# Two attention units of a batch in lockstep, in 64x32 and 32x64 tiles, with q, k, v read in long runs and the first phase's weights split on GpSimd

## The chip, the cores and the metric

One core of a Trainium2 chip runs the whole program in one launch. The metric is the device time of an execution in microseconds, the median over repeated runs. All inputs and outputs are float32 in HBM. TensorE (PE) multiplies, with its weight loads in a row of their own (PEld); VectorE (DVE), ScalarE (ACT) and GpSimd (POOL) do the rest; the DMA queues of SyncE (SP) and GpSimd bring the data.

## The reference

Three stages run one after the other, for a batch of 8 with 8 heads, 576 tokens and head width 64.

```python
def sm_attn(qq, kk, vv):                      # scale = 1/8
    s = scale * qq @ kk.T
    a = exp(s - max(s)); a = a / (sum(a) + 1e-9)
    return a @ vv
p_packed = sm_attn(p, k, v)                   # p: 32 rows per head
out      = sm_attn(q, p_packed, p_packed)     # 576 x 32 scores per head
x = out as (8, 576, 512)
# first phase: token shift, then
v = relu(xk @ w_k)**2 @ w_v ; r = sigmoid(xr @ w_r) ; x2 = r * v
# second phase: u = x2 + (x2.T @ U @ V).T ; result = u + relu(u @ w_ch1) @ w_ch2
```

## The kernel before

**Phases.** The 4608 rows of x are worked in two phases. In the first, four pairs of batches are done, each in three chunks of 384 tokens. A chunk has 17 slots (`SLOTS`): eight "k" slots (12 matmuls of 384 columns each, into `relu(x @ w_k)`), three "r" slots (12 matmuls of 512 columns) and six "v" slots (12 matmuls of 512 columns each). Each product is made in three passes over a high and a low float32r part, which ACT (high, a copy) and DVE (low, a subtraction) split off. In the second phase nine blocks of 512 tokens go through the 512 x 2048 x 512 network; the change leaves it alone.

**Attention.** A unit is four heads of a batch, so there are 16. A unit has ten steps ("k", "p", "scores1", "q", "a", "pv", "pp", "scores2", "norm", "out") that stand between the slots of the chunks. `chunk_plan` writes one list of items in order, and every engine and the SP queue walk that same list, each doing its own part of an item; so an engine that waits in one item does nothing of the next ones. `pair_units` says in which slot each step stands. The first pair works units 2 to 6 in its slots, the two middle pairs four units each (one hardware loop over both), the last pair one. Units 0 and 1 run before the first slot, in two sets of buffers, `main` and `side`, with the weights' staging between their steps (`first_items`).

**On the engines.** PE does two heads at a time: `scores1` and `scores2` are four matmuls of 288 columns with 128 rows and 64 output columns (L389, L417), because p and the packed result stand block-diagonally (`p_blk`, `pk_blk`, made with `mask`); `pv` is ten of 128 columns (L404), `out` four of 288 with 64 rows and 128 output columns (L425); `p`, `pp` are a transpose each and `a` five (L380, L409, L395). These are plain float32, and a matmul leaves two records in the profile. Between them stand DVE steps: two 32x32 transposes of k and two of q (L466, L473), a maximum, and for the second softmax transpose, maximum, subtraction, then sum, reciprocal, product and transpose (L489 to L507).

**What the first matmul of the chunks waits for.** `mix` and `split` of the first chunk need x of batch 0 from units 0 and 1, and in program order they stand behind all ten pieces of the phase's weights (L1098 on ACT, L1166 on DVE), which go through four staging buffers (`RA = 4`).

**Loads.** k comes in four DMAs a unit (two runs of 4480 bytes per partition), q in eight with runs of 128 bytes, v in sixteen with runs of 256 bytes. k and q are each loaded one unit ahead.

Of the kernel before, what the change touches and what calls it, by code (L numbers as in the profile page):

```python
# [26 lines left out]
P = 128  # L27
B, H, S, D = 8, 8, 576, 64
NP = 32
# [5 lines left out]
VLOADS = 16  # L35
# [17 lines left out]
T_STEPS = ("p", "a", "pp", "out1")  # L53
S_STEPS = ("scores1", "pv", "scores2", "out0")
NT, NS = len(T_STEPS), len(S_STEPS)
UNIT_STEPS = ("k", "p", "scores1", "q", "a", "pv", "pp", "scores2", "norm", "out")
# [10 lines left out]
RA, RB = 4, 3  # L67
# [4 lines left out]
WEIGHTS_AFTER = {"a": 2, "pv": 2, "pp": 1, "scores2": 2, "norm": 3}  # L72
# [4 lines left out]
def unit_slots(start, gaps=(0, 1, 2, 3, 4, 5, 6, 7, 8, 10, 11)):  # L77

    steps = (("k",), ("p",), ("scores1",), ("q",), ("a",), ("pv",), ("pp",), ("scores2",), ("norm",), (), ("out",))
    return {start + at: sum((own for gap, own in zip(gaps, steps) if gap == at), ()) for at in gaps}  # L80


def pair_units(kind):


    if kind == FIRST:
        early = {0: ("a",), 1: ("pv",), 2: ("pp",), 3: ("scores2",), 4: ("norm",), 6: ("out",)}
        return [(2, early), (3, unit_slots(7, (0, 1, 1, 1, 2, 3, 4, 5, 6, 7, 8))),
                (4, unit_slots(16)), (5, unit_slots(28)), (6, unit_slots(40, range(11)))]
    starts = {MIDDLE: (1, 14, 26, 38), LAST: (1,)}[kind]  # L90
    return [(3 + j, unit_slots(start)) for j, start in enumerate(starts)]


def chunk_plan(c, kind):
# [6 lines left out]
    late = kind == FIRST and c == 0  # L101
    for at, slot in enumerate(SLOTS):
# [8 lines left out]
        for n, plan in pair_units(kind):  # L111
            steps = plan.get(s, ())
            items += [("attn", n, step) for step in steps]
            if kind != LAST:
                if "k" in plan.get(s - 1, ()):
                    items.append(("load_k", n + 1))
                if "q" in plan.get(s - 1, ()):
                    items.append(("load_q", n + 1))
                if "pv" in plan.get(s - 1, ()):
                    items.append(("load_pv", n + 1))  # L120
# [10 lines left out]
        if not last_chunk:  # L131

            at0 = (12, 13, 14, 15) if c == 0 else MIX_AT
            where = dict(zip(at0, (("mix", 0), ("split", 0), ("mix", 1), ("split", 1))))
            if late:

                where = {9: ("mix", 0, 1, (0,)), 10: ("split", 0, 1, (0,)), 15: ("mix", 0, 1, (1,)),
                         16: ("split", 0, 1, (1,))}
            if at in where:
                items.append(where[at][:2] + (c + 1,) + where[at][3:])  # L140
        if kind == FIRST and c == 1 and at == 0:
            items += [("mix", 1, 1), ("split", 1, 1)]
# [10 lines left out]
def first_items():  # L153
# [3 lines left out]
    for step in UNIT_STEPS:  # L157
        items += [("attn", 0, step), ("attn", 1, step)]
        if step == "k":
            items.append(("load_k", 2))  # L160
        if step == "q":
            items.append(("load_q", 2))
        if step == "pv":
            items += [("load_pv", 2), ("u_prep",)]
        for _ in range(WEIGHTS_AFTER.get(step, 0)):
# [3 lines left out]
    items += [("attn", 2, "k"), ("mix", 0, 0), ("attn", 2, "p"), ("split", 0, 0), ("attn", 2, "scores1"),  # L169
              ("attn", 2, "q"), ("load_k", 3), ("load_q", 3)]  # L170
# [33 lines left out]
def main_ordinal(n):  # L204

    return 0 if isinstance(n, int) and n == 0 else n - 1


class Lane:


    def __init__(self, sb, sem, tag, scope):
        def buf(name, shape):
            return sb(name + tag, shape, F32, scope)
# [3 lines left out]
        self.kz, self.qz = buf("k_parts", [P, 2, KB * D]), buf("q_parts", [P, 2, KB, 32])  # L218
# [1029 lines left out]
```

## Time and profile before

| | |
|---|---|
| median of 3 runs | 1520.62 us (1519.82 to 1520.99) |
| the profiled execution | 1520.71 us |
| its span in the profile | 1518.4 us |
| first matmul of the chunks | 73.64 us into the span |
| share of PE's span with a matmul | 95% |
| DVE, ACT, POOL | 38%, 29%, 2% |
| mean granted TensorE clock | 0.982 |

The span leaves out some 2 us at the ends of an execution. Of PE, DVE and ACT a row gives the time of one instruction; on PE the instructions are pipelined, so the time of one (say 390 ns) is longer than the distance between two (some 230 ns), and the chain of work tells more: it follows the work that ended last back through time, so the pieces it lists add up without overlap.

### The profile page before, as it was taken

How to read it: one execution, taken by the hardware profiler on the slowest of the kernel's cores; microseconds unless marked ns; L12 is line 12 of the kernel's file. 1: busy time of each engine (PE TensorE's matmuls, PEld its weight loads, DVE VectorE, ACT ScalarE, POOL GpSimd, SP SyncE). 2: the span in 40 equal slices, each digit the busy share in tenths (PEclk: the TensorE clock that was granted, in tenths of full speed). 3: DMA queues.
4: the chain of work that ended last, by engine and by line, in shares of the span. 5: the costliest groups of instructions: out<-in, count | busy, mean ns of one | idle time of the engine just before them, and what ended most of it. 6: DMA issues, size and time to landing. Idle time of an engine off the chain costs nothing.

```text
span 1518.4 us, 18053 instructions
## 1 busy us (share of the span) xinstructions
PE 1449.3 (95%) x7048; PEld 1194.2 (79%) x7048; DVE 579.6 (38%) x933; ACT 442.9 (29%) x766; POOL 29.6 (2%) x65
## 2 busy tenths in 40 slices
PE   3289999999999999999999999999999999999999
PEld 1177788888878878888888888888888888888887
DVE  3655766666666666535221221212112121121211
ACT  2353554554455445434211111111111111111110
POOL 5000000000000000000000000000000000000000
PEclk9599999999999999999999999999999999999999
DMA  9533343343233310035110010100101010010000
GB/s 212 148 70 76 77 90 77 80 84 84 69 88 72 87 46 20 21 104 182 52 55 8 0 63 0 63 1 15 48 0 63 1 57 6 1 56 0 29 0 28
DMA packets 144127, 84.90 MB, mean 56 GB/s; under 512 B 115440, under 2 KB 119696, under 8 KB 144048
## 3 DMA queue, kind: packets, MB, share of 16 engines
q1 hardware_dynamic: 142960, 82.51, 20.9%
q0 software_dynamic: 1088, 1.33, 0.5%
q8 instruction: 49, 0.80, 0.2%
q14 instruction: 30, 0.25, 0.1%
HBM read 63.36 MB, written 20.45 MB: 55 GB/s over the span
## 4 chain that ended last, share of the span: by engine, by line
PE 91%; DVE 3%; SPq 3%; issue 1%; ACT 1%; DMA 1%; DVEq 0%; ACTq 0%
PE bank L1058 26%; PE bank L1028 26%; PE bank L578 19%; PE bank L612 12%; SPq L823 1%; PE bank L678 1%; PE bank L404 1%; SPq L834 1%; PE bank L745 1%; PE bank L425 1%; PE bank L417 1%; PE bank L389 1%; DVE mixed L553 1%; PE bank L749 1%; PE bank L1044 1%
## 5 line engine op out<-in xcount | busy, mean ns | idle before, releaser
L1208 DVE SCALAR_TENSOR_TENSOR hid_lo<-bank,hid_hi 128x512 fp32r<-128x512 f32 x144 | 99.6, 692 | 499.3 <-ACT hid_hi L1138 499.3
L1138 ACT ACTIVATE hid_hi<-bank 128x512 fp32r<-128x512 f32 x144 | 86.1, 598 | 599.7 <-PE bank L1058 599.7
L1058 PE MATMUL bank<-uT_hi,w_hi 128*128 128x512 f32 x576 | 224.9, 390 | 0.0
L1058 PE MATMUL bank<-uT_hi,w_lo 128*128 128x512 f32 x576 | 224.4, 390 | 0.0
L1058 PE MATMUL bank<-uT_lo,w_hi 128*128 128x512 f32 x576 | 224.4, 390 | 0.0
L1028 PE MATMUL bank<-w_hi,hid_lo 128*128 128x512 f32 x576 | 224.2, 389 | 0.0
L1028 PE MATMUL bank<-w_hi,hid_hi 128*128 128x512 f32 x576 | 224.1, 389 | 0.0
L1028 PE MATMUL bank<-w_lo,hid_hi 128*128 128x512 f32 x576 | 224.1, 389 | 0.0
L578 PE MATMUL bank<-xk_hi,wk_hi 128*128 128x384 f32 x384 | 133.6, 348 | 3.7 <-DVE xk_lo L570 3.7
L578 PE MATMUL bank<-xk_lo,wk_hi 128*128 128x384 f32 x384 | 130.2, 339 | 0.0
L578 PE MATMUL bank<-xk_hi,wk_lo 128*128 128x384 f32 x384 | 130.2, 339 | 0.0
L1058 PEld LDWEIGHTS bank<-uT_hi,w_lo 128*128 128x128 f32 x576 | 108.1, 188 | 22.7
L1028 PEld LDWEIGHTS bank<-w_hi,hid_lo 128*128 128x128 f32 x576 | 108.1, 188 | 22.5
L1028 PEld LDWEIGHTS bank<-w_hi,hid_hi 128*128 128x128 f32 x576 | 108.1, 188 | 22.5
L1028 PEld LDWEIGHTS bank<-w_lo,hid_hi 128*128 128x128 f32 x576 | 108.1, 188 | 22.3
L1058 PEld LDWEIGHTS bank<-uT_hi,w_hi 128*128 128x128 f32 x576 | 108.2, 188 | 21.8
L1058 PEld LDWEIGHTS bank<-uT_lo,w_hi 128*128 128x128 f32 x576 | 108.2, 188 | 21.6
L612 PE MATMUL bank<-wv_hi,k_hi 128*128 128x512 f32 x288 | 115.5, 401 | 0.0
L612 PE MATMUL bank<-wv_lo,k_hi 128*128 128x512 f32 x288 | 112.6, 391 | 0.0
L612 PE MATMUL bank<-wv_hi,k_lo 128*128 128x512 f32 x288 | 112.4, 390 | 0.0
L652 DVE TENSOR_TENSOR square<-square 128x384 f32<-128x384 f32 x96 | 53.0, 552 | 94.8 <-ACT square L632 94.6
L578 PEld LDWEIGHTS bank<-xk_hi,wk_hi 128*128 128x128 f32 x384 | 73.2, 191 | 13.9 <-issue 11.2
(152 smaller groups left out, 1722.0 us busy)
## 6 DMA issues: line engine op xcount, KB each, us to landing
k_parts<-in_k SPq DMA_DIRECT2D x60, 280.0 KB, 4.9
x_scratch<-x SPq DMA_DIRECT2D x36, 256.0 KB, 2.0
x_b<-x_scratch SPq DMA_DIRECT2D x9, 1024.0 KB, 6.2
out_dram<-x_b SPq DMA_DIRECT2D x36, 256.0 KB, 2.0
q_parts<-in_q SPq DMA_DIRECT2D x120, 72.0 KB, 2.3
x_b<-in_moe_w_ch SPq DMA_DIRECT2D x16, 512.0 KB, 3.9
v_rows<-in_v SPq DMA_DIRECT2D x120, 40.0 KB, 1.9
v_rows<-in_v SPq DMA_DIRECT2D x120, 32.0 KB, 1.8
```

What stands on the lines that cost most here:

```text
L389: last = nc.tensor.matmul(L.reg_s[rows, h * 512:h * 512 + HALF], L.pT[:, rows], L.kT[:, j, h * HALF:(h + 1) * HALF], start=True, stop=True)
L404: last = nc.tensor.matmul(L.reg_s[rows, 0:2 * D], L.aT[:, t * P + j * 2 * NP:t * P + (j + 1) * 2 * NP], L.vn[:, 2 * j:2 * j + 2, t, :], st ...
L417: last = nc.tensor.matmul(L.reg_s[rows, h * 512:h * 512 + HALF], L.pkT[:, rows], L.qT[:, j, h * HALF:(h + 1) * HALF], start=True, stop=True)
L425: last = nc.tensor.matmul(reg[:, h * 512:h * 512 + HALF], L.pk_blk[rows, :], L.aT[rows, h * HALF:(h + 1) * HALF], start=True, stop=True)
L553: last = nc.vector.scalar_tensor_tensor(out3, segments(c, ft, 0), mu[:, which, ft:ft + 1], out3, ALU.mult, ALU.add)
L578: last = nc.tensor.matmul(bank, a, b_, start=(done == 0), stop=(done == 3 * n_terms - 1))
L612: last = nc.tensor.matmul(bank, k2[a][:, f, at * P:(at + 1) * P], wv[b_][:, f, :], start=(f == 0 and a == 0 and b_ == 0), stop=(f == NFA - ...
L652: nc.vector.tensor_tensor(square[:, at % 2, :], square[:, at % 2, :], square[:, at % 2, :], ALU.mult).then_inc(squared, 1)
L1028: last = nc.tensor.matmul(acc[t], hid[a][:, f % RH, t * P:(t + 1) * P], w2s[b][:, f, :], start=False, stop=(f == NFB - 1 and a == 1))
L1058: last = nc.tensor.matmul(bank, w1s[a][:, ct, f * P:(f + 1) * P], uT[C % 2][b][:, ct, :], start=(ct == 0 and a == 0 and b == 0), stop=(ct ...
L1138: nc.scalar.activation(hid[0][:, f % RH, :], h_bank[(NFB * C + f) % 3], ACT.Relu).then_inc(h_hi, 1)
L1208: nc.vector.scalar_tensor_tensor(hid[1][:, f % RH, :], h_bank[(NFB * C + f) % 3], 0.0, hid[0][:, f % RH, :].bitcast(F32), ALU.max, ALU.sub ...
```

## The change

Units are gone; a batch's eight heads are worked together, in thirteen steps ("kA", "kB", "p", "scores1", "qA", "a", "qB", "pv", "pp", "scores2", "norm", "outA", "outB"). In detail:

- `scores1` and `scores2` are sixteen matmuls of 288 columns with 64 rows and 32 output columns (`L.reg[hp]` by row half, `quarter(c)` of its partitions); `outA` and `outB` are eight each, with 32 rows and 64 output columns; `pv` is forty of 64 columns with 128 rows and 32 output columns; `a` is ten transposes and `pp` one. The transpose of p on PE, `mask` and the block-diagonal tiles are gone: GpSimd scales p, DVE transposes it.
- k and q go through one buffer of two slots (`ZS = 2`), in eight parts a batch (`KQ`), four DMAs each of one run of 4480 bytes per partition. Parts 2, 3 (k) and 4 to 7 (q) are asked for only when the two before them have been turned by DVE. In batch 0 all eight have a place of their own. v comes in six DMAs, with runs of 1024 and 256 bytes; p in four.
- DVE turns each part of k in two instructions (the order of the tokens in the output is changed on the way), of q in one; its work on the softmaxes is the same, twice per batch in a row instead of once per unit. The last transpose writes its output with a stride of 18 elements.
- In batches after the first, the steps stand 0, 2, 3, 4, 5, 7, 8, 9, 11, 13, 17 and 19 slots after the first of them. Batch 1 fills slots 0 to 9 of the first pair, batches 2 and 3 begin in its slots 14 and 31; each middle pair has two that begin in slots 2 and 26; the last pair has none.
- The low parts of the first phase's weights are made by GpSimd instead of DVE, with three staging buffers instead of four; the ten pieces stand later in the list. The first chunk's `split` for r waits for all of them.
- The middle pairs are written out instead of looped over.

```diff
-WEIGHTS_AFTER = {"a": 2, "pv": 2, "pp": 1, "scores2": 2, "norm": 3}
+WEIGHTS_AFTER = {"qB": 2, "pp": 2, "scores2": 2, "norm": 2, "outB": 2}
-RA, RB = 4, 3
+RA, RB = 3, 3
+def batch_slots(start, gaps=(0, 2, 3, 4, 5, 7, 8, 9, 11, 13, 17, 19)):
+    steps = (("kA",), ("kB", "p"), ("scores1",), ("qA",), ("a",), ("qB",), ("pv",), ("pp",), ("scores2",), ("norm",),
+             ("outA",), ("outB",))
...
+        early = {0: ("scores1",), 1: ("qA", "a"), 2: ("qB", "pv"), 3: ("pp",), 4: ("scores2",), 6: ("norm",),
+                 8: ("outA",), 9: ("outB",)}
+        return [(1, early), (2, batch_slots(14)), (3, batch_slots(31))]
+    return [(2, batch_slots(2)), (3, batch_slots(26))] if kind == MIDDLE else []
...
+LOADS_AFTER = {"kA": ("load_z", 0, 1), "kB": ("load_z", 0, 2), "qA": ("load_z", 0, 3), "qB": ("load_z", 1, 0),
+               "p": ("load_p", 1), "pv": ("load_v", 1)}
...
+    items += [("mix", 0, 0), ("split", 0, 0), ("attn", 1, "kA"), ("load_z", 1, 1), ("attn", 1, "kB"), ("load_z", 1, 2),
+              ("attn", 1, "p"), ("load_p", 2)]
...
             for h in range(2):
-                for j in range(2):
-                    rows = slice(j * 2 * NP, (j + 1) * 2 * NP)
-                    last = nc.tensor.matmul(L.reg_s[rows, h * 512:h * 512 + HALF], L.pT[:, rows],
-                                            L.kT[:, j, h * HALF:(h + 1) * HALF], start=True, stop=True)
+                for c in range(CT):
+                    for hp in range(2):
+                        last = nc.tensor.matmul(L.reg[hp][quarter(c), h * 512:h * 512 + HALF],
+                                                L.pT[half_of(hp), c, :],
+                                                L.kqT[half_of(hp), c, h * HALF:(h + 1) * HALF], start=True, stop=True)
...
+            for hp in range(2):
+                for t in range(TT):
+                    for c in range(CT):
+                        last = nc.tensor.matmul(L.reg[0][quarter(c), half_of(hp)],
+                                                L.probs[:, hp, t * P + c * NP:t * P + (c + 1) * NP],
+                                                L.vn[:, 2 * c + hp, t, :], start=(t == 0), stop=(t == TT - 1))
...
+            for c in range(CT):
+                for hp in range(2):
+                    last = nc.tensor.matmul(L.reg[c // 2][half_of(hp), c % 2 * 512:c % 2 * 512 + HALF],
+                                            L.pk[quarter(c), hp, :],
+                                            L.kqT[quarter(c), hp, h * HALF:(h + 1) * HALF], start=True, stop=True)
...
+        if isinstance(C, int) and C == 0 and which == 1:
+            act.wait_ge(w_lo, NWA)
...
+                nc.vector.transpose(L.kqT[:, hp, :].rearrange("p (i m) -> p m i", m=KB),
+                                    blocks(L.probs[:, hp, 0:S])).then_inc(L.a2T_ok, 1)
...
-        with eng.Fori(1, PAIRS - 1) as g:
+        for g in range(1, PAIRS - 1):
...
+        for quad in range(4):
+            hp, dh = quad // 2, quad % 2
+            src = (k if i < CT else q)[n, 2 * (i % CT) + hp, :, :].rearrange("(i m) d -> i (m d)", m=KB)
+            eng.dma_start(part[32 * quad:32 * quad + 32, 0:KB * D - 32],
+                          src[:, 32 * dh:32 * dh + KB * D - 32]).then_inc(done, 16)
...
+            eng.wait_ge(att.kq_ok, ZS if n == 1 and part == 0 else KQ * n + 2 * part)
+            for i in range(2):
+                load_z(eng, n, 2 * part + i)
...
+        for i in range(NWA):
+            _, dst, a = w_chunks[i]
+            pool.wait_ge(w_hi, i + 1)
+            nc.gpsimd.tensor_tensor(dst[1], parts(stage_a[:, i % RA, :], a), dst[0].bitcast(F32),
+                                    ALU.subtract).then_inc(w_lo, 1)
```

## Rows read from the trace of the kernel before

**Rows 1.** The page: busy time of each engine over the span

```profile
PE 1449.3 (95%) x7048; PEld 1194.2 (79%) x7048; DVE 579.6 (38%) x933; ACT 442.9 (29%) x766; POOL 29.6 (2%) x65
```

**Rows 2.** Stretches: length, PE, PEld, DVE, ACT, POOL busy; clock, DMA share, GB/s

```profile
40.00:60.00 20.00, 0.00 (x0) 0.00 (x0) 10.30 (x14) 6.54 (x7) 0.71 (x1) 0.50 0.74 205
73.60:139.40 65.80, 58.01 (x301) 46.69 (x302) 38.16 (x67) 28.70 (x50) 0.80 (x2) 0.93 0.33 72
139.40:247.10 107.70, 106.70 (x576) 86.86 (x577) 71.78 (x124) 56.36 (x102) 2.16 (x3) 0.98 0.37 81
247.10:556.80 309.70, 307.88 (x1675) 252.43 (x1674) 198.72 (x345) 155.29 (x281) 4.01 (x8) 1.00 0.35 79
```

**Rows 3.** Start of the kernel, in order of time: start, busy, what

```profile
1.00 1.80 SPq L813 DMA_DIRECT2D k_parts<-in_k  x4
8.69 1.44 DVE L466 STREAM_TRANSPOSE kT<-k_parts 128x576 f32<-128x576 f32 x2 [8.69 <-DMA k_parts<-in_k]
14.87 1.44 DVE L466 STREAM_TRANSPOSE kT_side<-k_parts_side 128x576 f32<-128x576 f32 x2 [4.75 <-DMA k_parts_side<-in_k]
30.60 11.34 SPq L823 DMA_DIRECT2D q_parts<-in_q  x8
68.16 2.13 ACT L540 ACTIVATE mixed<-x,one_minus_mu 128x384 f32<-128x384 f32 x4 [2.03 <-DVE x L512]
73.64 0.66 PE L578 MATMUL bank<-xk_hi,wk_hi 128*128 128x384 f32 x1 [0.94 <-DVE xk_lo L570]
```

**Rows 4.** The chain of work in the steady stretches: start, length, what

```profile
232.56 2.75 PE bank L612 x12
...
340.73 1.24 PE bank L404 x20
...
348.19 1.12 PE bank L417 x8
...
354.10 0.46 PE bank L678 x2
354.55 4.19 PE bank L578 x24
358.74 1.17 PE bank L425 x8
359.91 4.37 PE bank L578 x24
364.29 0.11 PE bank L380
...
366.97 1.12 PE bank L389 x8
```

**Rows 5.** Groups by line and form: count, busy, mean ns of one, idle before

```profile
L389 PE MATMUL bank<-kT_side,pT_side 128*64 128x288 f32 x8 | 2.1, 687 | 0.0
L389 PEld LDWEIGHTS bank<-kT_side,pT_side 128*64 128x64 f32 x8 | 0.9, 230 | 1.0 <-issue 1.0
L489 DVE STREAM_TRANSPOSE probs<-bank 128x576 f32<-128x576 f32 x15 | 11.7, 780 | 7.6 <-PE bank L417 7.6
L553 DVE SCALAR_TENSOR_TENSOR mixed<-x,mu,mixed 128x384 f32<-128x384 f32 x96 | 52.9, 612 | 26.0 <-ACT mixed L540 26.0
L652 DVE TENSOR_TENSOR square<-square 128x384 f32<-128x384 f32 x96 | 53.0, 552 | 94.8 <-ACT square L632 94.6
L972 POOL TENSOR_TENSOR p_blk<-mask,p_rows 128x128 f32<-128x128 f32 x15 | 8.1, 539 | 504.0 <-DMA p_rows<-in_p 503.9
L1098 ACT ACTIVATE wk_hi<-stage_a 128x1024 fp32r<-128x1024 f32 x4 | 4.2, 1053 | 3.9 <-DMA stage_a<-in_moe_w_k 3.9
L1166 DVE TENSOR_TENSOR wk_lo<-stage_a,wk_hi 128x1024 fp32r<-128x1024 f32 x4 | 4.7, 1210 | 0.0
```

**Rows 6.** DMA issues: count, KB each, median us from issue to landing

```profile
k_parts<-in_k SPq DMA_DIRECT2D x60, 280.0 KB, 4.9
stage_a<-in_moe_w_k SPq DMA_DIRECT2D x4, 512.0 KB, 4.8
```

More of the change, by code:

```diff
@@ L48 @@
 EPS = 1e-9
[L53 to L56, printed above, removed]
+UNIT_STEPS = ("kA", "kB", "p", "scores1", "qA", "a", "qB", "pv", "pp", "scores2", "norm", "outA", "outB")
 SLOTS = ([("k", f) for f in range(NFA)] + [("r", t) for t in range(TPC)]
@@ L398, in pe_attn @@
         elif step == "pv":
-            pe.wait_ge(L.t_sb, NT * n + 2)
+            pe.wait_ge(L.aT_ok, 2 * n + 2)
             pe.wait_ge(L.v_in, VLOADS * 16 * (n + 1))
-            for t in range(TT):
-                for j in range(2):
-                    rows = slice(j * 2 * NP, (j + 1) * 2 * NP)
-                    last = nc.tensor.matmul(L.reg_s[rows, 0:2 * D], L.aT[:, t * P + j * 2 * NP:t * P + (j + 1) * 2 * NP],
-                                            L.vn[:, 2 * j:2 * j + 2, t, :], start=(t == 0), stop=(t == TT - 1))
@@ L430, in act_attn @@
-    def act_attn(act, L, n, place, step, mixes):
-        b, quad = place
-        if step == "p":
-            act.wait_ge(L.t_ps, NT * n + 1)
-            nc.scalar.activation(L.pT[:, :], L.reg_t[:, 0:P], ACT.Copy, scale=SCALE).then_inc(L.t_sb, 1)
-        elif step == "scores1":
-            act.wait_ge(L.s_sb, NS * n + 1)
-            nc.scalar.activation(L.probs[:, 0:S].rearrange("p (a n) -> p a n", a=2), halves(L.reg_s), ACT.Exp,
-                                 bias=L.neg_max[:, :], accum_out=L.row_sum[:, :]).then_inc(L.exp1, 1)
+                for c in range(CT):
+                    for hp in range(2):
+                        last = nc.tensor.matmul(L.reg[hp][quarter(c), h * 512:h * 512 + HALF],
+                                                L.pkT[half_of(hp), quarter(c)],
+                                                L.kqT[half_of(hp), c, h * HALF:(h + 1) * HALF], start=True, stop=True)
@@ L440, in act_attn @@
+    def act_attn(act, n, slot, step, mixes):
+        L = att
+        if step == "scores1":
+            for hp in range(2):
+                act.wait_ge(L.max1, 2 * n + hp + 1)
+                nc.scalar.activation(L.probs[:, hp, 0:S].rearrange("p (a n) -> p a n", a=2), halves(L.reg[hp]),
+                                     ACT.Exp, bias=L.neg_max[:, hp:hp + 1],
+                                     accum_out=L.row_sum[:, hp:hp + 1]).then_inc(L.exp1, 1)
         elif step == "a":
-            act.wait_ge(L.t_ps, NT * n + 2)
@@ L446, in act_attn @@
+            nc.scalar.activation(L.pkT[:, :], L.reg[1][:, 0:P], ACT.Copy, scale=SCALE).then_inc(L.pkT_ok, 1)
         elif step == "scores2":
[L447 to L450 removed]
+            for hp in range(2):
+                act.wait_ge(L.sub2, 2 * n + hp + 1)
+                nc.scalar.activation(L.probs[:, hp, 0:S], L.probs[:, hp, 0:S], ACT.Exp).then_inc(L.exp2, 1)
+        elif step in ("outA", "outB"):
+            h = int(step == "outB")
+            act.wait_ge(L.out_ps, 2 * n + h + 1)
```

513 lines of the change are left out of this document (243 added, 270 removed).

## The prediction

> **What bounds the kernel now.** First the page: a matmul runs in 95% of the span, DVE is busy 38% and ACT 29% [rows 1]. Then the stretches, since the attention is only in the first 560 us. The two middle pairs take 309.7 us with a matmul in 307.9 of them at full clock, and DVE busy in 198.7, 64% [rows 2]: PE is the bound there and waits for nobody, so each us of PE work that goes is a us, until DVE or a load is late. Last the start, in order of time: the first chunk matmul comes at 73.64 us [rows 3], and from 40 to 60 us no matmul ran at all, with the DMA engines 74% busy [rows 2]. The first chunk has 58.0 us of matmuls in 65.8 us, the other two of the first pair 106.7 in 107.7.
>
> **PE work in a pair.** The chain of work gives the pieces [rows 4]. A k slot is 2.10 us (4.19 for two), an r or v slot 2.75, a pair of g matmuls 0.46. Three chunks are 3 x (8 x 2.10 + 9 x 2.75) + 9 x 0.46 = 124.7 + 4.1 = 128.8 us. A middle pair is 309.7 / 2 = 154.9, so four units cost 26.1 us, 6.5 a unit or 13.0 a batch. From the pieces: scores 1.12 twice, pv 1.24, out 1.17, a 5 x 0.11, p and pp 0.11 each, 5.4 together; the rest is what follows a change of tile shape, as the two k slots behind L425 that take 4.37 in place of 4.19. I put that at 0.2 us for each of the four tiled steps.
>
> **The new steps.** Each matmul leaves two records. At the start, at half clock, eight weight loads of 230 ns are busy for only 0.9 us in all [rows 5], so loads lie on each other in pairs; the eight matmul records take 2.1 us there and 1.12 in the steady state. Either two tiles work side by side, and a record streams its columns twice (288 columns x 2 at 2.4 GHz is 0.24 us, four rounds of two records 0.96), or the pair is the two passes of one matmul. I take tiles. Then eight tiles of 64x32 hold the sixteen matmuls of `scores1` in the same four rounds: 1.34 us a batch with the switch, in place of 2 x 1.34. `outA` and `outB` are two rounds each, 0.48 + 0.16 + 0.2 = 0.9, so 1.8 in place of 2.8. `a` stays at 1.1, one pp stays, the two p and one pp go (0.33). For `pv` there is no near row: forty matmuls leave 80 records with 80 weight loads. If four tiles always overlap it is as much streaming as 10 matmuls of 128 columns now, 1.24 + 0.2. If instructions come no faster than in L404 now (20 records and 20 loads in some 1.1 us, 27 ns each), it is 160 x 27 ns = 4.3 + 0.4 = 4.7. I take 2.9, about halfway. The same 27 ns would make a scores step (64 instructions) 1.7 + 0.4 and an out step 0.9 + 0.4. So a batch is 7.2 us at best, 12.7 at that rate, and 2.7 + 1.8 + 1.1 + 0.1 + 2.9 = 8.6 in my forecast, 4.4 less than 13.0.
>
> The Trainium skill ("TensorEngine Tiling (Array Packing)", Instruction Overhead) says that each matmul carries about 60 cycles whatever its width, and warns against tiling a dimension that is already small; `pv` goes from 128 to 64 columns. As an estimate from it, 80 records of 25 ns would be 2.0 us, within the bounds above; no row here shows so short a matmul.
>
> **DVE, ACT, loads in the steady slots.** DVE does the same transposes, maxima and products, in lumps twice as long: scores2 is 6 x 0.78 = 4.7 us, norm about 5.7 (0.75 + 0.18 + 0.27 + 0.76 + 0.78 and gaps, twice). A k slot needs 2 x 0.55 = 1.1 us of DVE in 2.1; `mix` is 4 x 0.61 [rows 5]. Three places where I find PE waiting in a middle pair:
> - Parts 2 and 3 of k are asked for once kA is turned. Four DMAs of 280 KB land 4.9 us after issue at 0.45 us an issue [rows 3, 6], so the last of as many bytes lands 6.2 us after the request. kA in slot 2 is done 2.8 us after PE is through that slot; then 6.2, half a us for the last turn, 0.8 more for its second half and p: 10 us, where scores1 stands 6.3 + 0.5 us on. PE waits 3.1 us, once a pair (the batch at slot 26 has r and v slots there, in which DVE waits for nothing, and 8.3 us).
> - scores2, split, norm and the v products of the batch at slot 2 fill DVE from slot 13 on: the third x2 product comes 14.5 us after scores2, and the next chunk's third k slot wants its bank at 12.5 to 13.6. 1 us.
> - The batch at slot 26 has scores2 and norm in k slots 3 and 5: r2 wants the last relu, which waits behind norm. 1.4 us.
>
> So 5.5 us a middle pair. The pair is 128.8 + 2 x 8.6 + 5.5 = 151.5, 3.4 less than 154.9; the two give 6.8. If PE's part gets slower these waits shrink; if it gets faster they grow. The last pair loses its unit: 6.5. What DVE gains from the weights' low parts gone to GpSimd (10 x 1.21) is in the start.
>
> **The start.** Before, k (1.12 MB) was turned at 8.69 us, the side lane's at 14.87, with v already running beside it [rows 3]; the same 2.3 MB of batch 0's k now come first and alone: 13 us. p, scores1, two maxima, two exponentials, ten transposes, copies and pv at half clock bring it to 24. v (1.2 MB) and all of q (2.3 MB, twice what q was, but 32 DMAs' issue of 0.45 where 8 of q cost 11.3 us [rows 3]) land behind k at 28, and DVE's pv waits for the q turn. The first three weight pieces come behind q, at 29 to 32. From there three staging buffers turn around: 4.8 us to land [rows 6], 1.05 on ACT [rows 5], and GpSimd's subtraction. GpSimd's nearest row is 0.54 us for 128 columns; 1024 are between DVE's 1.21 and 8 x 0.54 = 4.3 us. I take 2.8, in the middle. A turn is 8.7 us for three pieces, so the seven others take some 20, and 4 us more because batch 1's first k parts and v stand before them in the queue: the last high part at 55.5. Then mix and split, 5.5 us as now from 68.16 to 73.64 [rows 3]: the first chunk matmul at 61, 12.6 us earlier. At 1.21 it would be 57, at 4.3 some 65.
>
> The Trainium skill ("GPSIMD Engine Reference", Elementwise — side-by-side cycle accounting) has 4497 ns for an add of 2048 float32 against 2293 on the Vector engine; half of it is an estimate of 2.2 us, with which the start would come some 2 us sooner. It speaks for leaving such work on DVE, but DVE waits for the loads here.
>
> **The first pair.** Batch 1 is now worked in slots 0 to 9 with only two k parts loaded ahead, and PE, DVE and ACT all stop in list order behind it. k parts 2 and 3 land 6.2 us after kA: scores1 waits 4.7 us behind the first k slot. q's two loads come after each other, 6.2 us each: `pp` waits 2.8. scores2's lump and mix hold split for r: 5.0. norm behind it holds outA: 2.9. With 3.5 us of half clock the chunk is 128.8 / 3 + 8.6 + 18.9 = 70.4, 4.6 more than 65.8. The other two chunks have a whole batch each: 2 x (42.9 + 8.6 + 2.4) = 107.8, as before.
>
> **Sum.** -12.6 (start) + 4.6 (first chunk) + 0 - 6.8 (middle) - 6.5 (last pair) = -21.3 us. The span of 1518.4 becomes 1497.1; with the 2.3 us around it 1499.4 against 1520.71 for the profiled execution, which stands 0.1 over the median. I say 1499.
>
> **The rivals.**
> - *More overlap.* All tiled steps at their streaming time (7.2 a batch, 1.4 less, seven times 10) with half of it taken by DVE, and a start 4 us sooner: 1490. For it: the pairs in [rows 5]. 14 in 100.
> - *Instructions at 27 ns.* 12.7 a batch is +4.1 seven times, 29 us, less 10 of waits that are then hidden: 1518. For it: nothing here comes quicker; against: the loads that lie on each other. 10 in 100.
> - *Waits twice as long.* The two-slot buffer and the DVE lumps cost double, 2 x 5.5 + 4.8 + some 4 in the first chunk, 20 us: 1519. For it: DVE at 64% with lumps of 5 us between k slots; against: three banks of slack. 12 in 100.
> - *No more than two at a time, slower.* In the small tiles still only two records overlap: a scores step is 32 x 0.12 + 0.4 = 4.3, an out step 2.3, pv 2.6, 17 a batch. That is 8.4 more seven times, 59 us, less 12 of hidden waits: 1546. For it: [rows 5] shows two, never more, and could be one matmul's two passes. It ends slower from a batch of about 13 us on. 9 in 100.
> - My forecast: 55 in 100, own range 1491 to 1509.
>
> The range, 1483 to 1523, leaves out the fourth rival and about 8 in 100 at the ends. About 3 us (0.2%) is what a measurement here can tell: faster 0.80 (forecast, more overlap, most of the second and third rival's lower halves), same 0.07, slower 0.13.
>
> **What would show it.** The first matmul of the chunks at 61 and chunk 1 starting near 131; in the chain, scores pieces of 1.1 to 1.2 for a whole batch and pv between 1.3 and 4.5; middle pairs of about 151 us; PE waiting on kT's successor or p in one place a pair; GpSimd's 1024-column subtraction at 2 to 3 us. The prediction is wrong if the scores steps take over 3 us, if DVE's strided transpose is far from 0.78, or if the two-slot loads land later than 6 us.

## The result, and the profile after

| | median of its runs | lowest to highest | profiled execution | its span | mean granted clock |
|---|---|---|---|---|---|
| before | 1520.80 us | 1519.82 to 1524.20 | 1520.71 us | 1518.4 us | 0.982 |
| after | 1539.84 us | 1539.08 to 1544.92 | 1540.1 us | 1538.3 us | 0.981 |

The ratio is 1.0128, with a 95% interval of 1.0101 to 1.0155. The change makes the kernel slower by 19 us (1.3%); 21.8 us less was forecast, and the range ended at 1523. The forecast has the wrong sign.

The first line of the page, engine by engine, answers to [rows 1]:

```profile
PE 1414.1 (92%) x7728; PEld 1175.6 (76%) x7728; DVE 579.5 (38%) x939; ACT 427.0 (28%) x734; POOL 35.4 (2%) x36
```

PE is busy for less time than before (1414.1 against 1449.3 us), in a longer span. So PE's work did go away, and what was added is time in which PE stands. Where it stands, the stretches show. The first line is 40 to 60 us, as in [rows 2]; the others run from the first matmul of one stretch to that of the next: the first chunk, the other two of the first pair, the two middle pairs (start:end length, busy time and records of PE, PEld, DVE, ACT, POOL, then the clock, DMA share and GB/s):

```profile
40.00:60.00 20.00, 2.53 (x32) 0.67 (x32) 12.18 (x16) 7.46 (x9) 11.12 (x7) 1.00 0.80 191
70.90:150.40 79.50, 56.63 (x396) 46.24 (x397) 43.17 (x78) 28.06 (x51) 0.53 (x1) 0.83 0.36 91
150.40:276.30 125.90, 105.63 (x797) 86.48 (x796) 79.60 (x139) 57.10 (x99) 1.75 (x2) 0.93 0.41 102
276.30:584.10 307.80, 291.68 (x2014) 243.35 (x2013) 202.32 (x353) 147.22 (x265) 2.40 (x5) 0.98 0.34 87
```

Beside [rows 2]: PE was busy in 106.7 of 107.7 us of chunks two and three, and is busy in 105.6 of 125.9; in the middle pairs it was 307.9 of 309.7 and is 291.7 of 307.8. The middle pairs shed 16.2 us of PE work and gained 14.3 us of standing still. The first chunk comes at 70.89 and not at 61.

| part of the span | before | forecast | after | after less forecast |
|---|---|---|---|---|
| to the first chunk matmul | 73.6 | 61.0 | 70.9 | +9.9 |
| first chunk | 65.8 | 70.4 | 79.5 | +9.1 |
| chunks two and three | 107.7 | 107.8 | 125.9 | +18.1 |
| two middle pairs | 309.7 | 303.0 | 307.8 | +4.8 |
| last pair and what follows | 961.6 | 954.9 | 954.2 | -0.7 |

(The forecast's last row is its span of 1497.1 less the others.) The waits of PE in these three stretches, grouped by who ended them (total us, times, longest), first chunk first:

```profile
PE bank L611 <- DVE xr_lo L603: 12.5, 1, 12.5
...
PE bank L385 <- DVE pT L498: 5.5, 1, 5.5
PE bank L408 <- DVE packed L511: 4.8, 1, 4.8
...
PE bank L711 <- DVE x2s_lo L722: 14.3, 3, 5.1
PE bank L385 <- DVE pT L498: 2.9, 2, 1.5
...
PE bank L385 <- DVE pT L498: 9.1, 2, 4.9
PE bank L611 <- DVE x L696: 4.1, 2, 2.1
```

There are two kinds. `pT` and `packed` are what DVE does next after it has turned the second parts of k and of q: a load stands behind them. `xr_lo` and `x2s_lo` are DVE's own list: the split for r, and the split of the products that the g matmuls want. The chain of work shows what a load costs, at the end of the first chunk and in the second, for batch 2 (start, length, what):

```profile
146.38 0.34 SPq L846
...
149.54 3.52 DMA kq_parts<-in_k
153.09 0.71 DVE kqT L484
153.96 0.31 SPq L846
...
158.40 3.10 DMA kq_parts<-in_q
161.53 0.79 DVE kqT L488
...
169.00 0.78 DVE kqT L488
...
171.35 0.33 PE bank L408
```

Two parts are asked for when DVE has turned the two before them. From the request at 153.96 to the start of the next turn at 161.53 are 7.6 us: SP's eight issues at 0.42 us or more, then 3.1 us of transfer. The request at 146.38 is answered 6.7 us later, at 153.09, and the last round, to the turn at 169.00, is 6.7 us too. Three such rounds stand in a batch (k's second two parts, q's first, q's second), and the chain has no PE in it from 146 to 171. In the first middle pair the round for k's second two parts is 7.4 us:

```profile
285.84 0.34 SPq L846
...
289.01 4.23 DMA kq_parts<-in_k
293.27 0.71 DVE kqT L484
```

Behind the rounds of batch 2 comes the other kind:

```profile
177.77 0.79 DVE probs L516
...
186.17 2.21 DVE mixed L584 x4
...
190.38 1.26 DVE kqT L539
...
194.62 1.82 DVE xk_lo L603 x2
197.79 1.47 DVE mixed L584 x3
200.65 1.12 PE bank L711 x2
```

The eight heads' maxima, the first mix, the norm's transposes, a split and the second mix follow each other on DVE and ACT, and the g matmuls (L711) wait for the products behind them.

PE's new steps are about as short as the forecast's best case. From the chain in a middle pair, and from the first pair for L416 and L429:

```profile
366.60 1.13 PE bank L385 x32
...
373.40 1.09 PE bank L393 x10
...
382.98 1.25 PE bank L402 x80
...
176.53 1.22 PE bank L416 x32
...
208.09 0.76 PE bank L429 x16
```

### The profile page after: what moved, and what is told of

It reads as the page before. It is cut to its first block, busy times and chain, and to the rows that moved or that the text cites. A ratio compares the mean times of both kernels' runs of the same rounds, so it can differ in the third digit from the quotient of the medians.

```text
span 1538.3 us, 18150 instructions
## 1 busy us (share of the span) xinstructions
PE 1414.1 (92%) x7728; PEld 1175.6 (76%) x7728; DVE 579.5 (38%) x939; ACT 427.0 (28%) x734; POOL 35.4 (2%) x36
## 3 DMA queue, kind: packets, MB, share of 16 engines
q1 hardware_dynamic: 56048, 92.60, 21.8%
## 4 chain that ended last, share of the span: by engine, by line
PE 79%; DVE 9%; DMA 4%; SPq 4%; issue 2%; ACT 1%; POOL 1%; DVEq 0%; ACTq 0%
PE bank L1088 26%; PE bank L1058 25%; PE bank L611 13%; PE bank L645 10%; SPq L846 3%; DMA kq_parts<-in_k 1%; PE bank L778 1%; DMA kq_parts<-in_q 1%; DVE mixed L584 1%; PE bank L711 1%; DVE kqT L539 1%; DMA stage_a<-in_moe_w_r 1%; DMA stage_a<-in_moe_w_k 1%; DVE probs L535 1%; DVE tok_max L519 1%
## 5 line engine op out<-in xcount | busy, mean ns | idle before, releaser
L611 PE MATMUL bank<-xk_hi,wk_hi 128*128 128x384 f32 x384 | 134.8, 351 | 15.6 <-DVE xk_lo L603 11.5
L611 PE MATMUL bank<-xk_lo,wk_hi 128*128 128x384 f32 x384 | 131.9, 343 | 0.0
L611 PE MATMUL bank<-xk_hi,wk_lo 128*128 128x384 f32 x384 | 131.6, 343 | 0.0
L611 PEld LDWEIGHTS bank<-xk_hi,wk_hi 128*128 128x128 f32 x384 | 74.8, 195 | 25.8 <-issue 16.1
L665 ACT ACTIVATE square<-bank 128x384 f32<-128x384 f32 x96 | 47.0, 490 | 158.9 <-PE bank L611 134.5
```

Source lines behind the costliest of these rows:

```text
L611: last = nc.tensor.matmul(bank, a, b_, start=(done == 0), stop=(done == 3 * n_terms - 1))
L665: nc.scalar.activation(square[:, at % 2, :], bank[:, 0:CHUNK], ACT.Relu).then_inc(k_ev, 1)
```

## The experiments

All are edits of the kernel after. The table splits each profiled span in the same way as above; the starts of the chunks are the first matmuls of L611 or its successor. Each row of stretches is one profiled execution: starts that no edit touches lie between 70.9 and 72.3 us (after, e1, e2, e5, e6), and middle pairs that none touches between 307.8 and 309.0, so a us or so in one stretch tells nothing. A ratio is taken to runs of the kernel before that were made beside it (medians 1520.8 to 1522.0).

| | start | first chunk | chunks 2 + 3 | middle pairs | rest | span | median us | ratio to before (interval) |
|---|---|---|---|---|---|---|---|---|
| before | 73.6 | 65.8 | 107.7 | 309.7 | 961.6 | 1518.4 | 1520.80 | 1 |
| after | 70.9 | 79.5 | 125.9 | 307.8 | 954.2 | 1538.3 | 1539.84 | 1.0128 (1.0101 to 1.0155) |
| e1_noload | 72.3 | 67.3 | 123.5 | 297.0 | 954.5 | 1514.6 | 1514.86 | 0.9951 (0.9935 to 0.9968) |
| e2_move | 71.8 | 84.1 | 114.4 | 309.0 | 953.6 | 1532.9 | 1531.99 | 1.0065 (1.0048 to 1.0081) |
| e5_noload_move | 71.4 | 70.0 | 104.6 | 295.6 | 953.8 | 1495.4 | 1497.33 | 0.9843 (0.9826 to 0.9859) |
| e3_pair | 73.5 | 83.1 | 134.1 | 318.9 | 953.0 | 1562.6 | 1564.70 | 1.0287 (1.0269 to 1.0304) |
| e4_wdve | 76.1 | 81.5 | 129.2 | 308.0 | 953.8 | 1548.6 | 1548.42 | 1.0171 (1.0154 to 1.0188) |
| e6_phase | 71.3 | 84.9 | 112.6 | 314.3 | 953.9 | 1537.0 | 1538.61 | 1.0106 (1.0084 to 1.0127) |
| e7_firstc | 72.8 | 70.2 | 128.3 | 308.1 | 952.9 | 1532.3 | 1533.54 | 1.0077 (1.0060 to 1.0094) |
| e8_best1 | 72.0 | 76.7 | 109.9 | 310.9 | 955.2 | 1524.7 | 1526.59 | 1.0034 (1.0018 to 1.0049) |
| e9_zs3 | 73.5 | 72.1 | 122.6 | 297.8 | 953.8 | 1519.8 | 1522.73 | 1.0014 (1.0002 to 1.0026) |
| e10_cont | 72.3 | 80.6 | 126.6 | 303.7 | 956.9 | 1540.1 | 1537.02 | 1.0103 (1.0089 to 1.0118) |
| e11_best2 | 72.5 | 75.6 | 109.9 | 307.8 | 953.7 | 1519.5 | 1519.55 | 0.9992 (0.9983 to 1.0001) |
| e12_best3 | 73.2 | 68.6 | 109.0 | 298.1 | 952.8 | 1501.7 | 1509.30 | 0.9925 (0.9913 to 0.9938) |

**Loads or DVE's list: e1, e2, e5.** e1 leaves out the loads of parts 2 to 7, six of the eight parts of k and q, from batch 1 on; parts 0 and 1, v and p are still loaded, and every instruction of PE, DVE and ACT stays:

```diff
-            dve.wait_ge(L.z_in[i % ZS], 64 * fills)
+            if n == 0 or i < ZS:
+                dve.wait_ge(L.z_in[i % ZS], 64 * (n + 1))
...
-        if n == B:
+        if n == B or (kind == "load_z" and part > 0):
```

> From batch 1 on, parts 2 to 7 of k and q are not loaded at all (DVE turns what lies in the buffer). This part of the input is left out; all instructions on PE, DVE and ACT stay. Theory L (the two-slot buffer: each pair of parts is asked for only when the last is turned, some 7.5 us of eight issues, landing and turn, three times a batch, and PE runs dry in k slots): chunks 1 and 2 of the first pair fall from 63.0 us to about 54, its first chunk from 79.5 to about 68, the first chunk of a middle pair from 55.2 to about 51, some 38 us in all: about 1502 us. Theory D (DVE's doubled lumps for scores2 and norm next to mix and split hold PE, the loads only fill time in which DVE would be behind anyway): 5 to 8 us, about 1533.

e2 moves batches 2 and 3 in the first pair, so that the maxima and the norm fall in k slots:

```diff
-        return [(1, early), (2, batch_slots(14)), (3, batch_slots(31))]
+        return [(1, early), (2, batch_slots(10)), (3, batch_slots(28))]
```

> Batches 2 and 3 of the first pair start in slots 10 and 28 in place of 14 and 31, so that kA to qB stand in r and v slots, in which DVE has little that PE waits for; scores2 and norm then stand in k slots 4 and 6, and mix and split have the r and v slots with the loads. Theory L: the load round trips are hidden behind long slots, chunks 1 and 2 fall from 63.0 to 53 to 55: 16 to 20 us off, about 1522. Theory D: the lumps in k slots hold PE at least as much, the chunks stay at 60 to 65: 1535 to 1544.

e5 is both edits together.

> The first two experiments together: parts 2 to 7 of k and q not loaded from batch 1 on (left out), and batches 2 and 3 of the first pair started in slots 10 and 28. If the load round trips and DVE's chain (scores2, mix, norm, split in the r slots) each hold chunks 1 and 2 by themselves, either alone gave little because the other was left, and both together take them from 63 to 50 to 52: about 1492 us. If the two gains only add up (25 and 8 us off 1539.8): about 1507.

The median falls by 25.0 us for the loads alone, by 7.9 for the places alone, and by 42.5 for both. In the first pair, which is where the places are changed, it is 14.6, 6.9 and 30.8 us: 9.3 more together than one by one. So neither theory stands alone: e1 and e2 both fall between their two forecasts, and e5's 1497.3 is nearer to the 1492 of two delays that hold the chunks each by itself than to 1507. The stretches of e5 (first chunk, chunks two and three, middle pairs):

```profile
71.40:141.40 70.00, 56.58 (x438) 45.61 (x439) 46.49 (x86) 31.35 (x58) 1.06 (x2) 0.90 0.19 44
141.40:246.00 104.60, 97.80 (x755) 81.11 (x754) 75.02 (x131) 48.09 (x89) 1.27 (x1) 1.00 0.26 63
246.00:541.60 295.60, 287.06 (x2014) 240.62 (x2013) 200.68 (x353) 145.99 (x264) 2.16 (x5) 1.00 0.16 44
```

In the second chunk the causes stand in for each other. Between the first matmuls of its k slots and of the next chunk's there are 63.0 us after the change (150.4 to 213.4), 63.1 without loads (139.6 to 202.7), 62.0 with the places moved (155.9 to 217.9), and 53.9 with both (141.4 to 195.3). The third chunk is another case: 62.9 us after the change, 60.4 in e1, 52.4 in e2 and 50.7 in e5, so there the places alone give nearly all; and e2 makes the first chunk 4.6 us longer, since batch 2 now begins in it four slots sooner. With the loads gone, the same wait for the products is left over, to the tenth of a us (after: 14.3, 3, 5.1, above), and the one for `pT` is 0.4 (e1, chunks two and three):

```profile
PE bank L712 <- DVE x2s_lo L723: 14.3, 3, 5.1
...
PE bank L385 <- DVE pT L499: 0.4, 1, 0.4
```

With the places moved and the loads kept (e2) it is the other way about: no wait for `x2s_lo` is left in these chunks, and one for `pT` has grown to 5.3:

```profile
PE bank L385 <- DVE pT L498: 5.3, 1, 5.3
```

With both gone no wait there is over 2.8 us. The middle pairs are 10.8 us shorter in e1. e2 doesn't touch them, and they stay as they were (309.0).

Part of the loss is the clock. After the change 162.3 us of matmuls stand in the first pair (56.6 + 105.6, 1193 records); in e5 it is 154.4 (56.6 + 97.8, also 1193 records), at a granted clock of 1.00 in the last two chunks against 0.93. The same work takes 7.9 us more. PE stands still for 43.1 us in the first pair after the change and for 20.2 in e5; the granted clock goes down to 0.50, the lower of its two levels (1.2 and 2.4 GHz), in the long waits and comes back only some us after them: it is 0.50 from 111.3 to 125.0 us, where PE waited from 108.8 to 121.3, and from 196.7 to 203.5, where it waited from 195.6 to 200.65. In the middle pairs the same work takes 4.6 us more than in e5 (291.7 less 287.1).

**Bytes or round trips: e3, e9.** e3 asks for two parts in four DMAs whose runs hold both, so a batch has half the round trips, each of twice the bytes:

```diff
-            for i in range(2):
-                load_z(eng, n, 2 * part + i)
+            for quad in range(4):
+                hp, dh = quad // 2, quad % 2
+                lo = hp + 4 * (part % 2)
+                src = (k if part < 2 else q)[n, lo:lo + 3:2, :, :].rearrange(...)
+                eng.dma_start(att.z[32 * quad:32 * quad + 32, :, 0:KB * D - 32],
+                              src[:, :, 32 * dh:32 * dh + KB * D - 32]).then_inc(att.z_in[0], 16)
```

> From batch 1 on two parts come in four DMAs with two runs of 4480 bytes per partition in place of eight DMAs with one; the same bytes. SP issues for 1.8 us in place of 3.7. Theory L: a round trip falls from 7.5 to about 6 us, three times in each of three batches of the first pair and once or twice in the middle ones: 8 to 15 us off, about 1528. If the transfer's rate bounds the round trip and not the issue (1.15 MB at some 230 GB/s is 5 us), 3 us or less. Theory D: no change.

It is slower, by 24.9 us, where each of the forecasts had it faster or unchanged. The chain of e3, and the DMA issues of after and of e3 (count, KB each, median us from issue to landing):

```profile
153.90 6.13 DMA kq_parts<-in_k
160.06 0.71 DVE kqT L484
161.64 0.31 SPq L881
...
164.02 5.42 DMA kq_parts<-in_q
169.46 1.45 DVE kqT L488 x2
```

```profile
kq_parts<-in_k SPq DMA_DIRECT2D x120, 140.0 KB, 3.2
```

```profile
kq_parts<-in_k SPq DMA_DIRECT2D x56, 280.0 KB, 5.2
```

A round is now 9.4 us from turn to turn (160.06 to 169.46), where it was 8.4 at this place (153.09 to 161.53), and no part can be turned before both have landed. Fewer issues don't help; the landing grows with the bytes, and it is on the path.

e9 leaves the transfers as they are and gives them a third slot, and asks for each part as soon as a slot is free. Its room comes from the squares, which lie where their low parts go, each in a place of its own and with the waits that they had:

```diff
-ZS = 2
+ZS = 3
...
-            fills = 1 if n == 0 else 2 + 4 * (n - 1) + i // 2
+            G = i if n == 0 else KQ * (n - 1) + i
+            fills = 1 if n == 0 else 2 + G // ZS
```

> Three slots for the k and q parts in place of two; a part is asked for as soon as its slot is free, so that one of the two parts that a step turns has been asked for a step earlier. Room for the slot comes from the squares, which stand in the place of their low parts. Nothing else moves. The loads' share by the run without them is 25 us (1539.8 against 1514.9). With a third slot a pair waits for some 5 us in place of 7.5, and half of that is asked ahead: 10 to 18 us off, about 1526; the first chunk of a middle pair from 55.2 to about 51. If the transfer rate is what bounds (all parts of a batch take 20 us in any case), 5 us or less.

17.1 us of the 25.0 that e1 gained come back with all bytes moved, within the 10 to 18 that were forecast. The middle pairs of e9:

```profile
268.20:566.00 297.80, 288.49 (x2014) 241.51 (x2013) 201.49 (x353) 146.17 (x265) 2.30 (x5) 0.99 0.35 88
```

297.8 us is within 0.8 of e1 (297.0), though the DMA engines are busy 35% here and 16% there. So there the transfers cost next to nothing by themselves: 10.0 of the 10.8 us were the turn of a buffer of two slots. In chunks two and three e9 has the same wait for the products as e1 (14.2 us in three).

**DVE's order in the first chunk: e7.** kA's turn goes ahead of the first mix, and the norm from slot 6 to slot 7, behind the split for r:

```diff
-        early = {..., 4: ("scores2",), 6: ("norm",),
+        early = {..., 4: ("scores2",), 7: ("norm",),
...
-    items += [("mix", 0, 0), ("split", 0, 0), ("attn", 1, "kA"), ("load_z", 1, 1), ("attn", 1, "kB"), ...
+    items += [("attn", 1, "kA"), ("load_z", 1, 1), ("mix", 0, 0), ("split", 0, 0), ("attn", 1, "kB"), ...
```

> Only batch 1's steps in the first chunk are moved: norm stands in slot 7, behind split for r, in place of slot 6 ahead of it; kA is turned before the first mix, so that parts 2 and 3 are asked for some 10 us sooner. PE waited 12.5 us for xr_lo and 5.5 for pT in this chunk. If these two orders are what makes the chunk 79.5 us where it was 65.8: 8 to 12 us off, about 1530. If the waits only move to the next step in the list (a2 after norm, the q parts): 3 us or less.

The first chunk goes from 79.5 to 70.2 us, which is what was forecast for it (70.4); it begins 1.9 us later, chunks two and three take 2.4 more, and the median falls by 6.3, less than the 8 to 12 of the expectation. PE's wait for the split in the first chunk of e7, 12.5 us before:

```profile
PE bank L611 <- DVE xr_lo L603: 6.1, 1, 6.1
```

**All softmax lumps in k slots: e6, e8, e11.** e6 puts every batch at slots 9 and 26 and takes outA and outB close behind the norm, in the middle pairs too:

```diff
-def batch_slots(start, gaps=(0, 2, 3, 4, 5, 7, 8, 9, 11, 13, 17, 19)):
+def batch_slots(start, gaps=(0, 2, 3, 4, 5, 7, 8, 9, 11, 13, 16, 17)):
...
+        return [(1, early), (2, batch_slots(9)), (3, batch_slots(26))]
+    return [(2, batch_slots(9)), (3, batch_slots(26))] if kind == MIDDLE else []
```

> Every batch after batch 1 starts in slot 9 or 26, so in the first r slot of a chunk, in the first pair as in the middle ones; outA and outB stand 16 and 17 slots after kA. That is the place of the batch at slot 26 of the middle pairs, around which chunks take 49 us in place of 55. If the place of the loads and of DVE's lumps against mix and split is what costs: chunks 1 and 2 of the first pair 50 to 53 in place of 63, the first chunk of a middle pair 49 to 51 in place of 55, some 28 us off: about 1512. If a batch costs its waits wherever it stands: 1535 or more.

e6 comes to 1538.6, so the 28 us are not there. The first pair gains 7.9 us (84.9 + 112.6 against 205.4), but the middle pairs lose 6.5: in a middle pair of e6 PE waits 7.0 us in two for the norm's turned tokens in front of outA (L429). So slots 9 and 26 are better for the first pair alone. e8 is e6 with e7's order and each part asked for as soon as its own slot is free:

```diff
-            eng.wait_ge(att.kq_ok, ZS if n == 1 and part == 0 else KQ * n + 2 * part)
             for i in range(2):
+                eng.wait_ge(att.kq_ok, ZS - 1 + i if n == 1 and part == 0 else KQ * n + 2 * part - 1 + i)
                 load_z(eng, n, 2 * part + i)
```

> The last two together, and each part of k or q asked for as soon as the part in its slot is turned, not the pair. The two edits are in different chunks and should add up: 28 and 10 us, and 1 us of each of some nine round trips: about 1497, below the kernel before (1521). If the waits only move: above 1521.

e11 is e8 with the middle pairs as the change has them.

> Batches 2 and 3 of the first pair from slots 9 and 26 with outA and outB 16 and 17 slots on, the middle pairs as in the change, batch 1's kA ahead of the first mix and its norm behind split for r, and parts asked for one by one. First pair 186 us (as in the run with all of this), middle pairs 153.5 in place of 155 to 158: about 1520, level with the kernel before.

e8 is 12.0 us faster than e6 but 30 above its forecast: the gains don't add up to 38. e11 is another 7.0 faster, of which the middle pairs have 3.1 in the traces (e8's ten times lie between 1521.79 and 1533.04, so the 7.0 is rough). e11 is level with the kernel before, as forecast: its interval reaches from 0.9983 to 1.0001.

**The start: e4.** DVE takes the weights' low parts again, GpSimd nothing:

```diff
-        for i in range(NWA):
-            _, dst, a = w_chunks[i]
-            pool.wait_ge(w_hi, i + 1)
-            nc.gpsimd.tensor_tensor(dst[1], parts(stage_a[:, i % RA, :], a), dst[0].bitcast(F32), ...
+            elif item[0] == "w":
+                i = item[1]
+                dve.wait_ge(w_hi, i + 1)
+                nc.vector.tensor_tensor(dst[1], parts(stage_a[:, i % RA, :], a), dst[0].bitcast(F32), ...
```

> DVE makes the low parts of the first phase's weights again, as before the change, in the list order of the change; still three staging buffers. A subtraction takes 1.22 us on DVE against 2.4 on GpSimd. If the turn of the staging buffers sets the first chunk matmul (70.9 us): 2 to 4 us sooner. If the transfers do (k and q of batch 0, the parts, v and p of batch 1 stand before the weights in the same queue), or DVE's waits for batch 0's steps hold the buffers: within 2 us of 1539.8, to either side.

The kernel gets slower by another 8.6 us, which neither expectation had; the first chunk matmul comes at 76.1, 3.8 to 5.2 us later than in the kernels whose start is that of after, and the first pair takes 5.3 us longer, for which the trace gives no cause. In e4's list on DVE both heads' norms of batch 0 (57.10 to 63.59 us) stand ahead of the last four low parts, which come at 63.43 to 71.92; after the change GpSimd has done them by 66.87. So the work on GpSimd is worth having. After the change, the group of the subtraction, and the start in order of time:

```profile
L1016 POOL TENSOR_TENSOR wk_lo<-stage_a,wk_hi 128x1024 fp32r<-128x1024 f32 x4 | 9.6, 2407 | 18.5 <-ACT wk_hi L1127 18.5
```

```profile
32.45 1.06 ACT L1127 ACTIVATE wk_hi<-stage_a 128x1024 fp32r<-128x1024 f32 x1 [10.07 <-DMA stage_a<-in_moe_w_k]
35.97 0.35 SPq L889 DMA_DIRECT2D stage_a<-in_moe_w_k  x1
...
43.57 1.06 ACT L1127 ACTIVATE wk_hi<-stage_a 128x1024 fp32r<-128x1024 f32 x1 [5.93 <-DMA stage_a<-in_moe_w_k]
...
63.39 1.06 ACT L1127 ACTIVATE wv_hi<-stage_a 128x1024 fp32r<-128x1024 f32 x1 [1.35 <-DMA stage_a<-in_moe_w_v]
70.89 0.66 PE L611 MATMUL bank<-xk_hi,wk_hi 128*128 128x384 f32 x1 [11.48 <-DVE xk_lo L603]
```

A piece asked for at 35.97 is split from 43.57 on, 7.6 us later, where 4.8 was taken from [rows 6]. The last high part stands at 64.4, not at 55.5. The chain of work names what lies on the path between these rows:

```profile
41.95 11.86 DMA stage_a<-in_moe_w_r
...
57.32 2.31 POOL wv_lo L1016
```

The sixth piece is asked for right behind the six DMAs of batch 1's v and takes 11.9 us to land. Of the 55 us from 20 to 75 the landings of weights have 27.2 us of this chain (11.57, 11.86 and 3.72) and GpSimd's subtractions 9.6, since a staging buffer is free only when its low part is made. GpSimd waits for ACT often (18.5 us in the group above), so it isn't short of time, but its 2.4 us are part of each turn.

**The strided transpose: e10.** The last transpose of the norm writes in one run; the tokens then stand in another order, which nothing mends.

```diff
-                nc.vector.transpose(L.kqT[:, hp, :].rearrange("p (i m) -> p m i", m=KB),
+                nc.vector.transpose(blocks(L.kqT[:, hp, :]),
```

> DVE's last transpose of the second softmax writes its 576 columns in a row in place of with a stride of 18 elements; the order of the tokens in the result is left unmended. The strided one took 1259 ns against 779 of the contiguous one before the change: 16 x 0.48 = 7.7 us of DVE, 1 us in each norm lump. Where PE waits for the lumps (first pair, scores2 and norm in r slots) the us goes through: 3 to 6 us off 1539.8. If the stride isn't what makes it long: no change.

After the change this transpose takes 1.26 us where the others of its size take 0.78 (count, busy, mean ns, idle before):

```profile
L539 DVE STREAM_TRANSPOSE kqT<-probs 128x576 f32<-128x576 f32 x16 | 20.1, 1259 | 0.6
```

In e10 it takes 778 ns, so the stride is what makes it long. Sixteen times 0.48 are 7.7 us of DVE; without them the median falls by 2.8, 0.2%, about what a measurement tells and just under the forecast of 3 to 6. The middle pairs are 4.1 shorter in the trace.

**Together: e12.** e11 and the third slot of e9. It has all loads and all work.

> The same with three slots for the parts. If the third slot's gain and the better places add up: 1507 to 1512, below the kernel before by 0.6 to 0.9%. If they are substitutes (with better places the loads are hidden already): 1518 to 1522.

```profile
73.20:141.80 68.60, 57.91 (x437) 46.31 (x438) 45.47 (x82) 31.66 (x58) 1.37 (x2) 0.93 0.49 121
...
250.80:548.90 298.10, 288.46 (x2013) 241.50 (x2012) 201.57 (x353) 146.13 (x264) 2.48 (x5) 0.99 0.35 88
```

1509.3 us, as forecast, 0.75% less than the kernel before and 2.0% less than after. Its five times run from 1503.57 to 1509.99, wider than other kernels here, and the trace is of the fastest; why is open. In that trace the first pair is 177.6 us, close to the 178.2 of the prediction, though with other slots than it assumed, and the middle pairs are 298.1, below its 303.0. Only the start is far from it (73.2 for 61.0).

## Why the prediction was wrong, point by point

**PE's work: right, and better than forecast.** A batch was put at 8.6 us with 7.2 as its floor. The scores steps take 1.13 and 1.22, an out step 0.76, `a` 1.09, and `pv`, the term with no near row, 1.25 where 2.9 was taken. Without loads (e5) the two middle pairs have 287.1 us of matmuls; the floor was 2 x (128.8 + 14.4) = 286.4. The rivals of 27 ns an instruction and of no more than two tiles at a time are both ruled out.

The Trainium skill ("TensorEngine Tiling (Array Packing)", Instruction Overhead) gives each matmul some 60 cycles, from which 2.0 us was estimated for `pv`. The estimate took the records one behind the other, and the trace doesn't agree with it: 80 records of matmuls in 1.25 us are 16 ns each, with 80 weight loads in the same time. They start in groups of four, one for each tile, 6 to 7 ns apart, and the groups some 56 ns apart; so one tile has 56 ns a record, and the trace doesn't speak against 60 cycles, 25 ns at 2.4 GHz, for each tile by itself.

**The step that failed, the largest: "The other two chunks have a whole batch each: 2 x (42.9 + 8.6 + 2.4) = 107.8, as before."** They take 125.9. Only waits of a middle pair were carried over, at 2.4 us a chunk. But the batches stand elsewhere in this pair: from slots 14 and 31 on, the maxima fall in slot 8 and the norm in slot 10 of a chunk, where the mixes, the splits and the products fill DVE's list too. In the first pair, 27.2 us over the forecast, moving them gives back 6.9 us, taking the loads away 14.6, and both 30.8. In the second chunk PE sees the longer of two delays, and the forecast had priced neither there. Its 2.4 us of waits a chunk were 4.8 in two; the trace has 20.3 us in which PE stands, 14.3 for the products, 4.8 for `pT` and `packed` and 1.3 for the norm. Another 5.4 us (105.6 of matmuls where 2 x (42.9 + 7.2) = 100.2 is the floor) go to the lower clock by estimate, which the sum had put at nothing there. Less the 2.8 that PE's steps were overpriced by, that is the 18.1.

**Round trips of the two-slot buffer, sized from one place.** The prediction had one wait per middle pair, 3.1 us, for k. It stands there, but the two `pT` waits of the middle pairs take 9.1 us, 4.6 each. The trip is 6.7 to 7.6 us and not 6.2: the sum took four DMAs of 280 KB, but the kernel issues eight of 140 KB, so the last one is issued only 3.2 to 4.4 us after the first and lands another 3.1 to 4.2 us later (and e3, which has the four DMAs of 280 KB, needs 7.8 from the request at 161.64 to the turn). The whole of it is 307.8 less 297.8 with a third slot, 10.0 us in two pairs, of which 3.2 are the same matmuls at a lower clock (291.7 less 288.5). All waits of these pairs are 16.1 us where 11.0 were forecast, and the lower clock takes 5.3 (291.7 less 286.4, an estimate) where the sum had nothing. With PE's own work 5.6 us less than forecast, the stretch was off by only 4.8: one error hid the other.

This is the rival "waits twice as long", with the right causes in its text ("the two-slot buffer and the DVE lumps"). It had 12 in 100, and its 1519 is still 21 us short. Over PE's own work at its floor the middle pairs have 307.8 less 286.4, 21.4 us of standing still and lower clock, where 11.0 of waits were forecast, so double; chunks two and three have 125.9 less 2 x (42.9 + 7.2), 25.7, where 4.8 was, five times as much.

**The first chunk: "scores2's lump and mix hold split for r: 5.0".** It was taken that the split for r comes ahead of the norm. In the list the norm of slot 6 stands ahead of the split that is added in the same slot, so PE waits 12.5 us. e7 puts them in the other order and the chunk takes 70.2 us, with 6.1 for that wait. It is no matter of loads: e5, without them, still waits 12.5. The two load waits in it are 5.5 and 4.8 us, where 4.7 and 2.8 were forecast, and outA doesn't wait for the norm at all (2.9 forecast): 22.8 us of waits for 15.4. The lower clock takes 6.5 by the same estimate (56.6 less 42.9 and 7.2) for 3.5.

**The norm's length, a sign that the prediction named.** The last transpose was put at 0.78 us and takes 1.26, so the lump is 6.4 us (188.38 to 194.78 in the chain) and not 5.7. scores2's lump was right, 4.6 for 4.7. By e10 the stride is worth 2.8 us of the whole, which is at the edge of what the runs can tell.

**The start: "the seven others take some 20, and 4 us more".** GpSimd's subtraction was sized well, 2.41 for 2.8 us. (The Trainium skill, "GPSIMD Engine Reference", Elementwise, led to an estimate of 2.2; the trace's 2.41 agrees within a tenth.) What was too short is the landing, 7.6 and 11.9 us for pieces for which 4.8 was taken. At that time batch 1's parts of k and its v are in the queues as well, and the DMA engines are 80% busy from 40 to 60 us at 191 GB/s, where the kernel before moved 205 [rows 2]. That the transfers of batch 1 lengthen it was not tried by itself, and neither was a fourth staging buffer, which the kernel before had, or another place for the pieces in the list; so the cause of the 9.9 us stays open between these. e4 shows only that with the subtractions on DVE the start is another 4 to 5 us later.

**The last pair: right**, 954.2 for 954.9.

The sum of the parts: 9.9 + 9.1 + 18.1 + 4.8 - 0.7 = 41.2, which is the whole of 1538.3 less 1497.1. Lockstep and small tiles are not what costs: e12 keeps them, with all of its loads, and is faster than the kernel before; the slots that the batches were put in and the buffer with two places are. No run has lockstep and tiles without the rest of the change, so their own worth isn't shown beyond PE's shorter work. In e12 the first chunk is still 68.6 us: 57.9 of matmuls and 10.6 of waits, 6.2 of them for the split for r. What each transfer costs in the start stays open.

## What to carry to other kernels

When steps are merged into longer ones, the matmuls' time is the easy part of the sum. Draw up each engine's list again in the new order, slot by slot, for every place where the merged step stands: the merged step needs a place where the other engines' lists are thin, and such a place in one stretch says nothing about another. A buffer that is asked for only when it has been turned puts a whole round trip, 6.7 to 7.6 us here, on the path once a turn, unless the other work between two turns is longer; a third place gave back 10.0 of 10.8 us in the steady stretches, with the same bytes moved. Two delays that run side by side may have to be taken away together before either shows: here each alone left the second chunk at 62 to 63 us, and both made it 53.9.

## What the hardware did that was not expected

- Matmuls in small tiles overlap. 32 records in 64x32 tiles, a whole batch, took 1.13 us at full clock, where 8 records of larger tiles took 1.12 for half of it [rows 4], and 80 records with 80 weight loads for `pv` 1.25 us.
- A transpose of 128x576 whose output has a stride took 1259 ns, and 780 ns [rows 5] with an output in blocks.
- With half as many load requests, each of 280 KB and not 140, a request landed 5.2 us after its issue and not 3.2, and the kernel was 24.9 us slower (e3, in which a turn also waits for both parts).
- A wait of PE costs more than its own length: in the first pair the same 1193 records took 162.3 us of busy time with 43.1 us of standing still among them and 154.4 with 20.2 (e5), at granted clocks of 0.83 and 0.93 against 0.90 and 1.00. So 22.9 us more of waits came with 7.9 us more of work.
